# Attention: in which order ScalarE takes the high part of tile c-1 and the exponential of tile c

## The reference, cut to what matters

```
batch, n_heads, seq, head_dim = (4, 8, 576, 64)
scores = scale * np.matmul(q, k.transpose(0, 1, 3, 2))
thresh = np.max(scores, axis=-1, keepdims=True) - tau
scores = np.where(scores >= thresh, scores, -1000000000.0)
scores = scores - np.max(scores, axis=-1, keepdims=True)
attn = np.exp(scores)
attn = attn / (np.sum(attn, axis=-1, keepdims=True) + 1e-09)
return np.matmul(attn, v).astype(np.float32)
```

## Time and profile before

| | us |
|---|---|
| median of 3 runs | 1315.62 |
| the profiled execution, its own time | 1315.53 |
| its span in the trace | 1313.8 |
| first and last exponential of the attention start at | 24.2 and 358.9 |
| TensorE busy with matmuls, whole span | 1244.9 |
| VectorE, ScalarE, GpSimd busy, whole span | 622.8, 539.4, 568.8 |

### The profile page before, as it was taken

The page is one execution under the profiler, slowest core; times in us unless marked ns, Lnnn a source line. Parts: engine busy times, 40 slices in busy tenths (PEclk is TensorE's granted clock), DMA queues, the critical chain, the costliest instruction groups (busy, mean ns, idle before and its releaser), DMA issues.

```text
span 1313.8 us, 20231 instructions
## 1 busy us (share of the span) xinstructions
PE 1244.9 (95%) x7678; PEld 1135.9 (86%) x7678; DVE 622.8 (47%) x1249; ACT 539.4 (41%) x966; POOL 568.8 (43%) x412
## 2 busy tenths in 40 slices
PE   5999999999885999999999999998999999999998
PEld 4899999989864889989999999997999999999997
DVE  7888888888745521212212121215544535444433
ACT  5777787878742243333333333333212112112111
POOL 5989999989810344343524434454511101000000
PEclk9999999999986999999999999999999999999999
DMA  5545454453520143343424333344221102000000
GB/s 174 129 120 139 125 148 125 128 135 100 168 52 25 57 153 111 130 129 96 132 93 144 101 123 125 105 161 128 82 73 49 32 1 73 16 0 24 16 1 25
DMA packets 71170, 123.14 MB, mean 94 GB/s; under 512 B 11824, under 2 KB 30512, under 8 KB 71088
## 3 DMA queue, kind: packets, MB, share of 16 engines
q1 hardware_dynamic: 57216, 86.90, 23.4%
q0 software_dynamic: 6080, 19.93, 4.9%
q10 hardware_dynamic: 7792, 15.21, 3.1%
HBM read 82.43 MB, written 19.92 MB: 78 GB/s over the span
## 4 chain that ended last, share of the span: by engine, by line
PE 79%; POOL 6%; issue 5%; ACT 4%; DVE 3%; DMA 2%; SPq 0%; ACTq 0%; POOLq 0%
PE h_ps L702 32%; PE y_ps L721 11%; PE y_ps L720 11%; PE y_ps L719 11%; PE o_acc L560 5%; POOL probs_lo L1311 4%; PE ring L530 2%; PE ring L531 2%; PE t_ps L680 2%; PE ring L544 2%; PE ring L543 2%; POOL k_parts L1316 1%; DMA k_parts<-k_ones 1%; ACT q_hi L805 1%; ACT probs_hi L797 1%
## 5 line engine op out<-in xcount | busy, mean ns | idle before, releaser
L702 PE MATMUL h_ps<-x_hi,region_a 128*128 128x384 f32 (+1 forms) x1408 | 343.8, 317 | 4.8 <-DVE x_lo L1203 4.3
L702 PEld LDWEIGHTS h_ps<-x_hi,region_a 128*128 128x128 f32 x1408 | 246.5, 189 | 11.6 <-DVE x_lo L1203 5.2
L1311 POOL TENSOR_TENSOR probs_lo<-probs,probs_hi 128x576 fp32r<-128x576 f32 x160 | 226.6, 1427 | 34.0 <-ACT probs_hi L797 34.0
L702 PE MATMUL h_ps<-x_lo,region_a 128*128 128x384 f32 (+1 forms) x704 | 221.2, 314 | 0.0
L1213 DVE SCALAR_TENSOR_TENSOR h_lo<-h_ps,h_hi 128x256 fp32r<-128x256 f32 (+1 forms) x128 | 62.8, 491 | 311.6 <-ACT h_hi L896 288.4
L899 ACT ACTIVATE h_hi<-act_out 128x384 fp32r<-128x384 f32 (+1 forms) x112 | 53.7, 480 | 312.3 <-DVE act_out L1224 305.8
L719 PE MATMUL y_ps<-region_b,h_hi 128*128 128x512 f32 x448 | 175.7, 392 | 1.4 <-DVE h_lo L1230 1.4
L720 PE MATMUL y_ps<-region_b,h_hi 128*128 128x512 f32 x448 | 176.5, 394 | 0.0
L721 PE MATMUL y_ps<-region_b,h_lo 128*128 128x512 f32 x448 | 176.5, 394 | 0.0
L1297 POOL TENSOR_TENSOR region_b<-stage,region_b 128x1024 fp32r<-128x1024 f32 x40 | 95.8, 2399 | 143.5 <-ACT region_b L778 143.4
L896 ACT ACTIVATE h_hi<-h_ps 128x256 fp32r<-128x256 f32 (+1 forms) x128 | 56.0, 437 | 240.2 <-PE h_ps L702 231.9
(11 more groups left out here) (202 smaller groups left out, 2406.3 us busy)
## 6 DMA issues: line engine op xcount, KB each, us to landing
stage<-in_moe_w SPq DMA_DIRECT2D x56, 512.0 KB
qk_raw<-in_qk SPq DMA_DIRECT2D x32, 320.0 KB, 3.4
expert_rows<-rows_out ACTq DMA_DIRECT2D x8, 768.0 KB, 3.9
v_nat<-in_v SPq DMA_DIRECT2D x16, 320.0 KB, 3.6
k_ones<-q_hi SPq DMA_DIRECT2D x30, 160.0 KB, 2.6
q_lo<-k_parts SPq DMA_DIRECT2D x30, 160.0 KB, 2.4
q_hi<-q_hi SPq DMA_DIRECT2D x30, 160.0 KB, 2.4
k_parts<-k_ones SPq DMA_DIRECT2D x30, 160.0 KB, 2.9
```

The lines of the kernel that those rows point to most:

```text
L702: mm = pe.matmul(h_ps[:, c % 2, 0:width], wt, x[kind][:, cc, :], start=(n == 0), stop=(n == 3 * C - 1))
L1311: pool.tensor_tensor(probs_lo[:, m % 4, :], probs[:, m % 4, :], probs_hi[:, m % 4, :].bitcast(F32), ALU.subtract).then_inc(lo_done, 1)
```

## The change

In every slot, high(c-1) now stands ahead of exp(c). Before, that was so only in the slot with j = 2; in the four others of a head it stood behind exp(c) and behind `q_hi` (j = 1) and `v_hi` (j = 4). No instruction is added or taken away, and no other engine's list changes.

```diff
@@ -796,8 +796,7 @@
                         wait(act, pv_done, tile(i, m) - 3)
                         act.activation(probs_hi[:, m % 4, :], probs[:, m % 4, :], ACT.Copy).then_inc(hi_done, 1)
 
-                if j == 2:
-                    high_parts()
+                high_parts()
                 exponentials()
                 if g is not None and has(i, g, NH, U):
                     wait(act, qk_in[g % U], (head(i, g) // U + 1) * 16)
@@ -815,8 +814,6 @@
                     wait(act, v_in[pair], (head(i, h - h % U) // U + 1) * 16)
                     wait(act, pv_done, tile(i, (h - 1) * NT))
                     act.activation(v_hi[:, lane, :, 0:D], v_nat[:, pair, lane, :, :], ACT.Copy).then_inc(v_hi_done, 1)
-                if j != 2:
-                    high_parts()
                 if j == 2 and has(i, c // NT - 1, NH, U):
                     h = c // NT - 1
                     if head(i, h) == 0:
```

## The result

| | us |
|---|---|
| kernel before, median of 5 runs | 1315.58 (1315.05 to 1317.46) |
| changed kernel, median of 5 runs | 1330.37 (1329.66 to 1332.53) |
| ratio | 1.0116, 95% interval 1.0102 to 1.0130 |
| profiled execution of the changed kernel, time and span | 1332.53 and 1330.7 |

The change made the kernel slower by 14.8 us; 17.1 us was forecast, and a time of 1332.6. The profiled execution is the slowest of the five.

The account below looks back on a forecast made before the run. TensorE was taken to set the pace, closely followed by GpSimd. Terms of 4.0 + 12.5 + 1 - 0.4 = +17.1 us on the profiled execution's 1315.53 us gave 1332.6 us, range 1320 to 1342.

Parts of the forecast that it names:

- The ring: Attention: exp, keep and high wait for each other in a closed circle, 2.13 us a turn, 159 steps; +4.0 us.
- VectorE at j = 3: Between keep(3) and keep(4) VectorE's copy, division and maxima take 2.56 us, 0.43 over a turn, in 29 heads; +12.5 us.
- The wait for TensorE: VectorE's 0.15 us wait for TensorE between keep(3) and keep(4) was expected to go, leaving 2.56 us of 2.71.
- ScalarE's other work: ScalarE's copies and eight weight pieces mostly fit into 0.99 us free per turn; bounds 0 to 5 us, taken as +1 us.
- the end: End of attention: the last low part comes about 2.2 us behind the last exponential instead of 2.69; -0.4 us.
- The waits counted at nothing: TensorE's 30.9 us of waits for low parts nearly vanish, but TensorE waits for VectorE's places instead; counted as 0.
- One sign: Waits of high parts for keep on ScalarE, 3 before, were to be near 160 and 25 to 40 us in total.
- The most loaded engine: Rival: TensorE, 95% busy, decides; 1300 us with half its low-part waits back, 1315.5 with none; chance 0.10.
- The ring without VectorE's long step: Rival: VectorE's j = 3 work finishes early and hides, so only +4.6 us remain; 1320 us, chance 0.12.
- The rival with TensorE in the ring at j = 4: exp(4) waits for TensorE's scores, keep(4) starts at 2.78 instead of 2.56 us; 6.4 us more, 1339 us; chance 0.14.
- The granted clock: Expected 1.00 in the attention; rival: TensorE's clock falls to 0.71, attention about 95 us longer, 1410 us, chance 0.02.
- whole durations: VectorE's j = 3 step, if each instruction waited for an empty pipe: about 0.15 us a head, 4 us more; not adopted.

Follow-up runs that it names:

- the first eight experiments: Changed kernel with old order in one slot (four), extra VectorE instruction (two), high not waiting for keep (one); the last also on the kernel before; 1290.73 to 1342.40 us.

## Why the prediction was right

**The ring (first term, +4.0 us).** Right as a mechanism, too large. The turn is 2.11, not 2.13 us: 159 x 2.11 = 335.5 against 334.7 is +0.8 us. The single turn that I read the earlier trace rows began with an exponential that had waited for TensorE; that one takes 0.65 us and hands over after 0.69. One that follows directly on a high part is recorded with 0.63, and keep starts 0.67 behind it (208.90 to 209.57 above).

**VectorE at j = 3 (second term, +12.5).** Right, slightly too small. The step is 2.60 and not 2.56, and a turn is shorter: 29 x (2.60 - 2.11) = 14.2 us. The wait for TensorE went away as forecast. The missing 0.04 lies ahead of the copy: it starts 0.85 us behind keep(3) (209.57 to 210.42), where rows 7 less the wait have 0.96 - 0.15 = 0.81. That it is on the path is shown from both sides: extra work in it counts in full, extra work at j = 2 not at all.

**ScalarE's other work and the end (+1, -0.4).** What is left of the 16.0 us is 16.0 - 0.8 - 14.2 = 1.0 us for the first of them, as taken. The trace shows it largely where the prediction put it. Of the eight weight pieces the two behind `q_hi` make the step to the next exponential 2.40 us instead of 2.11, here one of them, and the two behind `o_t` make it 2.15 and 2.16; one behind an exponential of j = 3 costs 0.03, and the other three nothing:

```profile
149.24 0.63 ACT L789 ACTIVATE probs<-ring 128x576 f32<-128x576 f32 x1
...
150.55 0.62 ACT L832 ACTIVATE region_a<-early 128x512 fp32r<-128x512 f32 x1
...
151.64 0.63 ACT L789 ACTIVATE probs<-ring 128x576 f32<-128x576 f32 x1
```

These add 0.7 us. The first head, with a piece and a slower TensorE at j = 3, adds 0.5, and the last head but one 0.1. That is 1.3 in all; the 0.3 too much is rounding, as the step behind j = 4 is 2.10 and not 2.11 in 29 heads. The last high part starts at 377.9 and the last low part at 378.7, 2.3 us behind the last exponential, against 2.69 before, as forecast.

**Sum.** The four terms at their measured sizes give 15.6 us; the medians differ by 14.8. The forecast of 17.1 is as near as it is partly by luck, as the first term was 3.2 us too large and the second 1.7 too small. That the profiled execution, at 1332.53, meets the forecast time to 0.1 us is luck altogether: its attention also began 1.5 us later than that of before, which is no term of the sum. From the last exponential to the end of the span it is 954.9 us in the profile of before, 954.3 in that of after, and 951.6 to 953.7 in those of the first eight experiments above, whose code there is the same. The first exponential starts at 24.2 before, 25.7 after, and at 24.6 to 26.0 in those. So single profiles differ by up to 3 us outside the changed stage, and the last microsecond can't be assigned.

**The waits counted at nothing.** TensorE's waits for low parts, 30.9 us before, are down to 6.1 us in 4 waits, all of them behind 360 us; two of these, 4.1 us, stand in the view of waits above as waits for `o_t` and under "issue". Waits for VectorE's places and for `o_t` took their place. What an order that avoids them can be worth is the 24 us between old and new order in the runs without the dependence.

**One sign was sized wrongly.** The prediction named 25 to 40 us of waits of high parts for keep, at nearly 160 high parts. They are 70.6 us at 127, since the high part behind `q_hi` and `v_lo` finds its keep done. The 0.17 us of the earlier trace rows was no measure of one wait, as another high part fills that gap. The prediction's own 0.99 us of free time in a turn, less the other work that ScalarE has in a head (0.73 + 0.24 + 0.64 + 0.59 + 0.46 = 2.66 us, rows of j = 1 to 4 in the profile of after), would have given 5 x 0.99 - 2.66 = 2.3 us a head, some 73 us in 32 heads. No term of the sum used this figure.

**The rivals.** The most loaded engine did not decide: a ring over two engines that are busy 78 and 80% of the stretch did (225.84 and 232.08 of 290 us). The Trainium skill, "Perfetto Trace Analysis", section "Identifying the Most-Contended Engine", says which engine to optimize first, and for TensorE it wants the busy share of the weight loads and not that of the matmuls. By either share TensorE came first before, at 265.31 and 275.87 of 290 us against GpSimd's 263.40. That an edit elsewhere is therefore free was the prediction's own step from there, and it would have been false. The ring without VectorE's long step, 1320 us, is refuted by the step of 2.60 us and by the extra work in it.

The rival with TensorE in the ring at j = 4 came close. exp(4) did wait 0.18 us for TensorE in each head (the row at 211.28 above), but it ended at 211.93, and VectorE was only free for keep(4) at 212.17. The granted clock was 1.00 from 34 to 365 us. In this profile it was 0.66 from 29 to 34 us and 0.57 from 374 to 378, with matmuls 0.24 us apart instead of 0.13; the first of these falls into the longer step of the first head, and the second delays no exponential.

VectorE's step did not come out longer by whole durations: the instruction of 0.75 us at 211.50 is again followed after 0.67. The Trainium skill, "VectorE: DVE Perf Modes", section "The DRAIN you can't avoid", from which the prediction took that the next instruction waits for an empty pipe, also says there that one that is not held starts earlier. These rows go with the second sentence.

## What to carry to other kernels

When an instruction moves ahead of another on one engine, ask whether what it waits for is started by the instruction that it is now behind. If so, a ring closes: its turn is the sum of its members' start-to-start times, engines that are 20% idle can then set the pace, and every longer step of a member engine is added instead of absorbed. Here it was enough to open the ring in one well-chosen slot per head, the one ahead of the longest step. Where the step is set by a member engine's own list, as at j = 4, opening the ring brought nothing.

## What the runs showed of the hardware

An activation that follows directly on another was recorded at 0.63 us, the same one after a wait at 0.65, and the engine reading its result followed 0.67 and 0.69 us after its start. Over 159 turns these 0.02 us are 3 us, so a turn should be read where every member runs as it will in the ring. VectorE's extra maximum, recorded with 0.54 us, made its step 0.43 us longer. Neither its recorded duration nor its own start-to-start time gives that: the next instruction started 0.55 us behind it, but 0.73 instead of 0.85 us behind keep stood the maximum itself, so that keep's own step became shorter by 0.12. At j = 2, in front of another instruction, its start-to-start time was 0.46 (206.89 to 207.35). The price of an instruction on a path is the growth of the whole step, and it depends on the neighbours.
